# Attention of two tiles at a time in every second expert half, w2's block sums and the q, k, v loads in other places

## The reference

```
attention: q, k, v (4 batches, 8 heads, 576 rows, 64 columns), in chunks of 64 rows:
    scores = q_c @ k_c.T / 8;  p = softmax(scores);  x = p @ v_c        -> x (2304 x 512)
gated layer:  a = x @ w_a;  b = x @ w_b;  x = (a * b) @ w_out            (512 -> 1536 -> 512)
experts:  p = probs / sum(probs)
          out = sum over e of p[:, e] * (relu(x @ w1[e]) @ w2[e])        (4 experts, 512 -> 1024 -> 512)
```

## Time and profile before

| | |
|---|---|
| median of 3 runs | 1175.73 us (1175.42 to 1176.02) |
| the profiled execution, its own time | 1175.47 us |
| its span, first to last instruction | 1173.7 us |
| TensorE (PE) busy | 1165.9 us, 99% |
| VectorE (DVE) busy | 859.4 us, 73% |
| ScalarE (ACT) busy | 502.6 us, 43% |
| DMA | 319.54 MB, mean 272 GB/s |
| granted TensorE clock | 0.999 of full |

### The profile page before, as it was taken

One profiled execution on the slowest core, in us unless ns is written; L12 is line 12 of the kernel. 1 busy time (PEld: TensorE's weight loads), 2 busy tenths in 40 slices (PEclk: granted clock), 3 DMA queues, 4 the chain that ended last, 5 costly groups with the idle time before them and its releaser, 6 DMA issues.

```text
span 1173.7 us, 18780 instructions
## 1 busy us (share of the span) xinstructions
PE 1165.9 (99%) x7604; PEld 1127.0 (96%) x7604; DVE 859.4 (73%) x1148; ACT 502.6 (43%) x868; POOL 0.7 (0%) x6
## 2 busy tenths in 40 slices
PE   9999999999999999999999999999999999999998
PEld 8999998888999899999999999999999999999998
DVE  6786889888887893367877777797346787777788
ACT  6554464445544542244544334334233533333334
POOL 0000000000000000000000000000000000000000
PEclk9999999999999999999999999999999999999999
DMA  7396885878987699939777777748894877776761
GB/s 271 139 345 238 299 323 215 330 304 329 349 310 269 259 414 362 329 133 340 297 265 260 281 280 259 248 163 285 251 359 168 340 262 262 253 264 249 265 250 75
DMA packets 73162, 319.54 MB, mean 272 GB/s; under 512 B 7340, under 2 KB 13812, under 8 KB 56692
## 3 DMA queue, kind: packets, MB, share of 16 engines
q1 hardware_dynamic: 72644, 317.56, 73.4%
q10 hardware_dynamic: 432, 0.79, 0.2%
HBM read 221.81 MB, written 96.51 MB: 271 GB/s over the span
## 4 chain that ended last, share of the span: by engine, by line
PE 92%; DVE 3%; DMA 2%; ACT 1%; issue 1%; SPq 0%; DVEq 0%; ACTq 0%
PE ps L682 30%; PE ps L684 30%; PE ps L683 30%; DMA kept_w<-w 1%; PE ps L691 1%; PE ps L710 1%; PE ps L699 1%; DMA kept_w<-lone 1%; PE ps L718 0%; PE ps L754 0%; DVE hw L1687 0%; ACT three L1117 0%; ACT hw L1117 0%; SPq L580 0%; DVE h L2032 0%
## 5 line engine op out<-in xcount | busy, mean ns | idle before, releaser
L1117 ACT ACTIVATE ps<-ps 128x384 f32<-128x384 f32 (+1 forms) x184 | 91.3, 502 | 198.4 <-PE ps L684 196.0
L682 PE MATMUL ps<-x,wab 128*128 128x384 f32 x504 | 169.2, 336 | 0.1
L684 PE MATMUL ps<-x,wab 128*128 128x384 f32 x504 | 168.4, 334 | 0.0
L683 PE MATMUL ps<-x,wab 128*128 128x384 f32 x504 | 168.4, 334 | 0.0
L1117 ACT ACTIVATE hw<-xraw 128x768 fp32r<-128x768 f32 x112 | 94.8, 847 | 139.6 <-DVE xraw L2170 58.5
L682 PE MATMUL ps<-x,w1s 128*128 128x384 f32 x448 | 152.0, 339 | 0.0
L682 PE MATMUL ps<-hw,w2s 128*128 128x384 f32 x448 | 151.0, 337 | 0.0
L684 PE MATMUL ps<-x,w1s 128*128 128x384 f32 x448 | 149.8, 334 | 0.0
L683 PE MATMUL ps<-x,w1s 128*128 128x384 f32 x448 | 149.8, 334 | 0.0
L684 PE MATMUL ps<-hw,w2s 128*128 128x384 f32 x448 | 149.8, 334 | 0.0
L683 PE MATMUL ps<-hw,w2s 128*128 128x384 f32 x448 | 149.8, 334 | 0.0
(11 more groups left out here) (202 smaller groups left out, 2251.8 us busy)
## 6 DMA issues: line engine op xcount, KB each, us to landing
wab<-kept_ab SPq DMA_DIRECT2D x70, 512.0 KB, 5.5
w1s<-kept_w SPq DMA_DIRECT2D x32, 1024.0 KB, 6.2
w2s<-kept_w SPq DMA_DIRECT2D x16, 2048.0 KB, 7.4
w1s<-kept_w SPq DMA_DIRECT2D x16, 1536.0 KB, 6.2
w2s<-kept_w SPq DMA_DIRECT2D x16, 1536.0 KB, 6.1
kept_ab<-wab SPq DMA_DIRECT2D x42, 512.0 KB, 5.8
raw<-in_w SPq DMA_DIRECT2D x16, 1024.0 KB, 10.3
kept_w<-w SPq DMA_DIRECT2D x16, 1024.0 KB, 12.8
```

Of the source, the lines that this page charges most:

```text
L682: pe.matmul(dst, stat(HI), mov(HI), start=first, stop=False, skip_group_check=True)
L683: pe.matmul(dst, stat(HI), mov(LO), start=False, stop=False, skip_group_check=True)
L684: return pe.matmul(dst, stat(LO), mov(HI), start=False, stop=last, skip_group_check=True)
L1117: return act.activation(dst, src, ACT.Copy)
```

## The change

TensorE scores two tiles in halves 0, 2 and 4 (the second one in columns 256 to 511 of the same banks), and transposes, and attends to, two tiles in halves 2, 4 and 6 (the second transposes go to bank 3). Odd halves hold none of it. The transposed p of these tiles goes into the place of the tile's own q in its slot. VectorE's `shift` of the second tile stands behind `split_w1(w+1, 0)`; `sum_w2` of halves 1, 3 and 5 goes to that place too. `normalise` stays one tile a half. ScalarE takes two exponentials at the start of halves 1, 3 and 5, and two `save_pT` and two `save_x` in halves 2, 4 and 6. SP loads q, k and v of tile 7 ahead of w2's stores of half 0 (and behind w1's); behind the block sums' stores it loads q and k of tiles 8 and 9 in half 0, v of 8 and 9 and q and k of 10 and 11 in half 2, and v of 10 and 11 in half 4.

```diff
         def slot_pT(t):
-            return pT_first[:, t % 2] if t < TILES else pT
+            return pT_first[:, t % 2] if t < TILES else slot(t, 0).rearrange("p (n c) -> p n c", n=4) if t < 2 * TILES else pT
+        def scored_by(w):
+            return min(2 * (w // 2 + 1), TILES)
...  first_windows (SP), behind the stores of w1
+                    if w == 0:
+                        sp.wait_ge(wot_kept, 64 * 3)
+                        load_qk(TILES + 1)
+                        load_v(TILES + 1)
...  behind load_w2(w + 1)
-                    if w == 0:
-                        sp.wait_ge(wot_kept, 64 * 3)
-                    if w + 1 < TILES:
-                        sp.wait_ge(scored, t)
-                        load_qk(t + 1)
-                        sp.wait_ge(attended, t)
-                        load_v(t + 1)
                     for u in ((w,) if w < 6 else (6, 7) if w == 6 else ()):
                         sp.wait_ge(wt_lo, 2 * u + 2)
                         sp.dma_start(kept_w2[u, :, 2:5], three[:, :].bitcast(F32)).then_inc(wt_kept, 16)
                         sp.dma_start(kept_w2[u, :, 0], lone[:, :].bitcast(F32)).then_inc(wt_kept, 16)
+                    if w == 0:
+                        sp.wait_ge(scored, t + 2)
+                        load_qk(t + 2)
+                        load_qk(t + 3)
+                    if w in (2, 4):
+                        sp.wait_ge(attended, t)
+                        load_v(t)
+                        load_v(t + 1)
+                    if w == 2:
+                        load_qk(t + 2)
+                        load_qk(t + 3)
...  first_part (TensorE)
-                            pe.wait_ge(shifted, w)
+                            pe.wait_ge(shifted, scored_by(w - 1))
-                    if s == 0 and w >= 2:
-                        pe.wait_ge(xf_set, TILES + w - 1)
+                    if s == 0 and w > 2:
+                        pe.wait_ge(xf_set, TILES + scored_by(w - 3))
...  second_part (TensorE)
-                if w < TILES:
+                if w in (0, 2, 4):
                     pe.wait_ge(h_lo, h_count(w, "C11", 1))
                     score(t, 0)
-                if 1 <= w <= TILES:
+                    score(t + 1, 0, 256)
+                if w in (2, 4, 6):
                     pe.wait_ge(t_set, 2 * Q + 2)
-                    turn_p(t - 1, 2)
+                    turn_p(t - 2, 2)
+                    turn_p(t - 1, 3)
-                    if i == 1 and 1 <= w <= TILES:
-                        attend(t - 1, 2)
+                    if i == 1 and w in (2, 4, 6):
+                        pe.wait_ge(pT_set, t)
+                        attend(t - 2, 2)
+                        attend(t - 1, 2, 256)
...  first_phase (ScalarE)
-                if 1 <= w <= TILES:
+                if w in (1, 3, 5):
                     exp(t - 1)
+                    exp(t)
-                if 1 <= w <= TILES:
-                    save_pT(t - 1, 2)
+                if w in (2, 4, 6):
+                    save_pT(t - 2, 2)
+                    save_pT(t - 1, 3)
-                if 1 <= w <= TILES:
-                    save_x(t - 1, 2)
+                if w in (2, 4, 6):
+                    save_x(t - 2, 2)
+                    save_x(t - 1, 2, 256)
...  shift (VectorE)
-            def shift(t, bank):
-                row_max(t, bank)
+            def shift(t, bank, at):
+                dve.wait_ge(scored, t - t % 2 + 2)
+                row_max(t, bank, at)
+                if t >= TILES + 2:
+                    dve.wait_ge(p_turned, t - 1)
...  first_phase (VectorE)
-                        sum_w2(w)
+                        if w % 2 == 0:
+                            sum_w2(w)
-                if w < TILES:
-                    shift(t, 0)
+                if w in (0, 2, 4):
+                    shift(t, 0, 0)
...  add_out(w, 0) and split_w1(w + 1, 0) stand here
+                if w in (0, 2, 4):
+                    shift(t + 1, 0, 256)
-                if w == 0:
-                    sum_w2(0)
+                if w in (0, 1, 3, 5):
+                    sum_w2(w)
                 add_out(w, 1)
```

More of the change, by code:

```diff
@@ L612, in later_windows @@
                 if T < NTH - 1:
-                    sp.wait_ge(scored, TILES * (T + 1))
+                    sp.wait_ge(attended, TILES * (T + 1))
                     load_qk(TILES * (T + 1))
@@ L700, in turn_p, with attend @@
                 last.then_inc(p_turned, 1)
-            def attend(t, bank):
+            def attend(t, bank, column=0):
                 pe.wait_ge(v_in[qk_slot(t)], 16 * loads(t))
@@ L708, in attend @@
                             rows = slice(BLK * u, BLK * (u + 1))
-                            at = m * P + BLK * b
+                            at = column + m * P + BLK * b
                             last = pe.matmul(ps[BLK * r:BLK * (r + 1), bank + u, at:at + BLK],
@@ L1134, in save_pT, with features @@
                 act.wait_ge(p_turned, t + 1)
-                if t >= 2:
-                    act.wait_ge(attended, t - 1 if t < TILES else t)
+                if 2 <= t < TILES:
+                    act.wait_ge(attended, t - 1)
+                elif t >= 2 * TILES:
+                    act.wait_ge(attended, t)
                 copy(slot_pT(t).rearrange("p n c -> p (n c)"), ps[:, bank, :]).then_inc(pT_set, 1)
-            def features(bank):
-                return ps[:, bank:bank + 2, 0:256].rearrange("p u (m c) -> p u m c", m=2)
+            def features(bank, at=0):
+                return ps[:, bank:bank + 2, at:at + 256].rearrange("p u (m c) -> p u m c", m=2)
             def round_x(t, bank):
@@ L1145, in round_x, with save_x @@
                 copy(x[:, blk:blk + 2, HI, :, at:at + P], features(bank)).then_inc(x_hi, 1)
-            def save_x(t, bank):
+            def save_x(t, bank, column=0):
                 T, at = t // TILES, t % 3 * P
-                if T:
+                if T == 1:
+                    act.wait_ge(attended, t - t % 2 + 2)
+                elif T:
                     act.wait_ge(attended, t + 1)
@@ L1154, in save_x @@
                 if t % TILES < 3:
-                    copy(xf(T)[:, (0 if T else 1):4:(3 if T else 2), :, at:at + P], features(bank)).then_inc(xf_set, 1)
+                    copy(xf(T)[:, (0 if T else 1):4:(3 if T else 2), :, at:at + P], features(bank, column)).then_inc(xf_set, 1)
                 elif T == 0:
@@ L1158, in save_x @@
                 else:
-                    copy(xf_at(T, F21)[:, :, at:at + P], features(bank)[:, 0])
-                    copy(xf_at(T, F22)[:, :, at:at + P], features(bank)[:, 1]).then_inc(xf_set, 1)
+                    copy(xf_at(T, F21)[:, :, at:at + P], features(bank, column)[:, 0])
+                    copy(xf_at(T, F22)[:, :, at:at + P], features(bank, column)[:, 1]).then_inc(xf_set, 1)
             def round_sum(T, a):
@@ L1698, in row_max @@
                 dve.wait_ge(max_set, t + 1)
-            def shift(t, bank):
-                row_max(t, bank)
-                dve.tensor_tensor(slot_p(t).rearrange("p (r n c) -> p r n c", r=2, n=4), scores_of(bank, 0),
+            def shift(t, bank, at):
[3 more added lines that the diff above has]
+                    dve.wait_ge(p_turned, t - 1)
+                dve.tensor_tensor(slot_p(t).rearrange("p (r n c) -> p r n c", r=2, n=4), scores_of(bank, at),
                                   by_head(rowmax[:, t % 2, :]).unsqueeze(3).to_broadcast([P, 2, 4, BLK]),
```

## The result

The changed kernel takes 1186.38 us (median of 6 runs, 1184.78 to 1187.24) against 1175.78 us for the kernel before in the same comparison: ratio 1.0088, 95% interval 1.0075 to 1.0101. It is slower by 10.6 us; 1185.5 was forecast. The profiled execution took 1185.13 us with a span of 1183.3 us, 9.6 us more than before. Half 7's first output product starts at 419.85 us against 410.26, so the whole difference lies ahead of it.

What follows compares the result with a forecast made beforehand. TensorE, 99% busy, bounds the kernel before; afterwards the loop through DMA and VectorE does. Its steps give T(6) = 371.0, plus 49.28 us to half 7 at 420.3, 10.0 us later: 1175.47 + 10.0 = 1185.5 us, range 1177 to 1191.

Steps and rivals of the forecast that it cites:

- The forecast's loop: Halves 1 to 5: block sums' stores, w1's load and stores landing, VectorE's serial work, next block sums' stores; sets the time.
- T(6): T(w) is when SP issues the stores of half w-1's block sums; T(6) forecast at 371.0 us, before 360.98.
- TensorE's stream: Small blocks of halves 0 to 6: pairing cuts 12.5 us to 10.4, 2.1 us shorter; 3.0 up to half 5's end.
- VectorE behind K: From K to the next block sums' stores: 12.6 us in odd halves with sum_w2 moved there, 11.4 in even ones.
- K: K(w): ScalarE starts overwriting w1 once its stores have landed; K(1) forecast near 222.4, K(3) 292, K(5) 358 us.
- The queue: Loads ahead of w1's stores in halves 1, 3, 5 cost 2.7, 4.05, 1.35 us, together 8.1, between nothing and double.
- B: Rival: the loads cost the stores nothing; 2.0 us late, 1177.5 us; chance 0.14.
- D: Rival: the loads run at half rate and cost double, 8.1 us more; 1189.5 to 1193.6, say 1191 us; chance 0.14.
- C: Rival: TensorE stays ahead and its shorter stream shows, half 7 starting 3.0 us sooner; 1172.5 us; chance 0.10.
- E: Rival: each second block of a pair costs 0.83 us, not 0.47; 2.2 us hidden in stalls, 1185.5 us; chance 0.05.
- The new wait for c: Inside halves 2, 4 and 6 TensorE waits about 2 us for add_c's result, as sum_w2 awaits late block-sum stores.
- The waits around them: TensorE waits 2 to 3 us at the starts of halves 2 and 4, forecast at 231.4 and 301.0 us.

Runs made afterwards that it cites:

- after_h: Changed kernel with its loads ahead of the block sums' stores and sum_w2 of halves 1 to 5 directly behind low_h: 1173.82 us, ratio 0.9984 to the kernel before.
- sum_early: Changed kernel with sum_w2 of the odd halves back ahead of low_h; pairs, second shifts and loads stay: 1177.73 us, ratio 1.0018 to the kernel before.
- loads_early: Changed kernel with q, k, v loads of halves 0, 2 and 4 ahead of the block sums' stores: 1177.10 us, ratio 1.0015 to the kernel before.
- half2_early: Changed kernel with only half 2's six loads moved ahead of the block sums' stores: 1182.41 us, ratio 1.0060 to the kernel before.
- b_loads_late: Kernel before with only its q, k, v loads moved behind the block sums' stores: 1176.01 us, ratio 1.0002.
- b_sum_mid: Kernel before with only sum_w2 of halves 1, 3 and 5 moved to the middle: 1175.88 us, ratio 1.0005.
- b_both: Kernel before, without pairs, with loads moved behind the block sums' stores and sum_w2 of halves 1, 3 and 5 in the middle: 1183.30 us, ratio 1.0068.
- both_early: Changed kernel with odd halves' sum_w2 back ahead of low_h and its loads ahead of the block sums' stores: 1175.92 us, ratio 1.0003 to the kernel before.

## Why the prediction was right

The forecast's loop and its place stood, and T(6) came within 0.5 us of the sum, in part by errors that cancel. By its own steps:

- *TensorE's stream* is shorter by what was read from single and neighbouring blocks; the pairs measured 2.12 and 1.30 us. The gain was covered by waits as said, and after_h shows that it was real.
- *VectorE behind K*: 12.6 us in odd halves was forecast; 12.59, 12.58 and 12.59 were measured in halves 1, 3 and 5 (the parts that the prediction lists add up to 12.66). sum_early shows the cause by taking it back.
- *The queue*: the loop was right and the size only roughly so. Over the distances that the sum took without loads (20.99, 20.5, 20.5), four, six and two loads cost 2.6, 3.5 and 0.6 us, together 6.6 where 8.1 was forecast. Moving the loads in the changed kernel gives 3.6 us for the four, 3.0 and 2.7 for the six (loads_early, half2_early) and 0.7 for the two. So the cost did not grow with the bytes as the sum had it. It is nearer the middle value than nothing (B) or double (D, 16.2), and both are out by this.
- *C*, TensorE staying ahead: not with this order. K(1) stood 24.8 us into half 1, which began near 197.1, beyond the 22.0 at which it decides, and TensorE waited. E is out by the pairs' rows.
- *The new wait for c*: 2.1 us in halves 2 and 4 was forecast, 2.07 and 2.03 were measured.
- *The waits around them*: half 4 was to start at 301.0 and did at 301.15, half 2 at 231.4 and did at 230.93. But of the 2 to 3 us that TensorE was to wait at the start of half 2 only 0.40 stood there; it had waited 1.94 us before, at the sixth output block of half 1, for an add_out behind K, a place that the forecast doesn't have. Ahead of half 4 only 0.43 us showed, as TensorE came to half 3 at 269.28 us in place of 267.9 (last section). And in half 6, where about 2 us for c were listed, it waited 0.26 us for c and 0.80 us for h. None of this moves the sum, because T(6) sets it.

Two terms were mis-sized, in opposite directions. Half 2's step was 1.15 us longer than forecast, and halves 3 and 5 together 1.4 us shorter (their 20.5 us and 4.05 or 1.35 from T to K were 0.6 and 0.8 too long). That they nearly cancel is luck: the 1.15 us are best explained by a low clock that the forecast did not have, and without it the step of half 2 was 32.04 us in half2_early (32.5 forecast). The forecast charged the loads and the sums to one loop with little slack, and b_loads_late, b_sum_mid and b_both show that each alone is harmless there and both together are not.

The expectations after it were less good where they followed a chain only to its first consumer: both_early missed the 1.55 us wait for low_h, which stands right behind sum_w2 in VectorE's program.

## What to carry to other kernels

When the busiest engine has no waits, find the loop with the least slack behind it. Here it is stores landing, then one engine's serial work, then the next issue. Before moving an instruction, ask on which side of the point where that loop's engine idles it will stand: sum_w2's 2.5 us were covered by VectorE's idle time ahead of K (6.50 us of it in half 1 of the changed kernel) and lengthened the loop by their whole length behind K. Two edits that each eat from the same slack must be costed together. If something waits for a store to land, loads put ahead of it in the same queue can delay it: here by 2.6 to 3.6 us for 1.05 MB. Place them where the queue is idle, and look at who waits for the loads themselves.

## What the runs showed of the hardware

After the 2.07 us wait in half 2 of the changed kernel, TensorE's products of 384 columns start every 0.32 us for a while in place of 0.173:

```profile
246.40 0.51 PE L695 MATMUL ps<-x,w 128*128 128x384 f32 x1
246.71 0.52 PE L696 MATMUL ps<-x,w 128*128 128x384 f32 x1
247.03 0.52 PE L697 MATMUL ps<-x,w 128*128 128x384 f32 x1
```

The windows of 3 us there give the granted clock in the third number from the end:

```profile
246.00:249.00 3.00, 3.00 (x12) 2.96 (x11) 2.98 (x7) 1.78 (x5) 0.00 (x0) 0.57 1.01 426
249.00:252.00 3.00, 3.00 (x76) 2.49 (x75) 2.65 (x5) 1.59 (x5) 0.00 (x0) 0.86 1.04 441
```

It is 0.57 of full on average from 246 to 249 us and 0.86 in the next window; 0.5 is the 1.2 GHz level. This happened once in that profile. Before it, TensorE had waited 1.94 us in half 1, 0.40 at the start of half 2 and 2.07 there. From the fourth product behind the wait to the scores pass 3.00 us (246.40 to 249.40); the same stretch in half 4, at full clock, takes 1.66, so the low clock cost 1.3 us there. I put the 1.15 us by which half 2's step exceeds the forecast down to TensorE's later arrival at the end of half 2, since that last low_wt stands behind the fifth output block. half2_early bears this out: it has the same waits up to there, 1.95, 0.44 and 2.00 us, its clock stayed at 1.00, and its step was 1.6 us shorter. In half 4 of the first profile, behind a wait of 2.03 us, the products kept their 0.173 us too. So like waits cost more than their length in one execution and not in another; what decides is open. The mean granted clock was 0.998 in five of the changed kernel's six executions and 0.999 in the sixth, against 0.999 or 1.0 in those of the kernel before that lie beside the experiments, so the low stretch was probably not in the profiled one alone. But the times don't follow it: the execution at 0.999 took 1186.67 us, and in half2_early the one at 0.998 was the fastest. The changed kernel's six times spread over 2.5 us, those of the kernel before beside them over 1.6.

The other thing is the queue. Where SP's stores of w1 set K, K stands 19.7 to 21.3 us behind T with no load ahead of them, 21.1 to 21.4 with two, 21.6 to 23.2 with three, 23.3 to 23.6 with four and 24.0 to 24.2 with six, taken over the ten profiles. Bytes over 389 GB/s gave the delay to 0.1 us for the four loads of half 0 against the kernel before, but 0.9 us too little against loads_early and 1.1 to 1.3 us too much for the six loads moved within the changed kernel. Why it is not proportional no run shows. The Trainium skill (DMA: Bandwidth & Descriptors, Queues, rings and completion order) says that an engine takes descriptors up in ring order. The runs agree in so far as loads issued ahead of the stores made them land later, and loads issued behind them did not.
